# Earlier and regrouped loads of q, k and v at the start of a kernel of attention and two MLPs

## The reference

```python
scores = cap * np.tanh(scale * (q @ k.T) / cap)
attn = np.exp(scores - max(scores)); attn = attn / (attn.sum() + 1e-9)
x = (attn @ v) reshaped to (896, 768)
x = square(relu(x @ w_in1)) @ w_out1        # w_in: 768 x 2048, w_out: 2048 x 768
x = silu(x @ w_in2) @ w_out2
```

## Time and profile before

| | |
|---|---|
| median of 3 runs | 555.83 us (555.57 to 556.46) |
| the profiled execution | 555.52 us, span 553.7 us |
| mean granted TensorE clock | 0.992 |
| PE busy | 537.8 us, 97% |
| DVE busy | 387.5 us, 70% |
| ACT busy | 258.9 us, 47% |
| POOL busy | 82.2 us, 15% |
| DMA | 42.16 MB, mean 76 GB/s |

### The profile page before, as it was taken

The page is one execution under the profiler, slowest core; times in us unless marked ns, Lnnn a source line. Parts: engine busy times, 40 slices in busy tenths (PEclk is TensorE's granted clock), DMA queues, the critical chain, the costliest instruction groups (busy, mean ns, idle before and its releaser), DMA issues.

```text
span 553.7 us, 7148 instructions
## 1 busy us (share of the span) xinstructions
PE 537.8 (97%) x2636; PEld 443.3 (80%) x2636; DVE 387.5 (70%) x621; ACT 258.9 (47%) x397; POOL 82.2 (15%) x54
## 2 busy tenths in 40 slices
PE   7999999999999999999999999999999999999994
PEld 5333333799988999999889999999999999998993
DVE  2189999977779653677799845556965255569983
ACT  3988889054444322444444444454432244443330
POOL 0989999300000000000000000000000000000000
PEclk9899999999999999999999999999999999999997
DMA  6679740151202202422012124111220141112544
GB/s 156 167 204 223 190 118 2 56 134 57 57 21 71 63 1 57 134 59 57 19 47 54 35 59 133 58 29 49 65 69 2 57 134 57 51 27 61 84 61 73
DMA packets 82372, 42.16 MB, mean 76 GB/s; under 512 B 27040, under 2 KB 79264, under 8 KB 82336
## 3 DMA queue, kind: packets, MB, share of 16 engines
q1 hardware_dynamic: 81184, 41.12, 28.8%
q10 hardware_dynamic: 1120, 0.57, 0.5%
q0 software_dynamic: 32, 0.00, 0.0%
HBM read 38.93 MB, written 2.75 MB: 75 GB/s over the span
## 4 chain that ended last, share of the span: by engine, by line
PE 84%; DVE 5%; SPq 3%; ACT 3%; DMA 1%; issue 1%; ACTq 0%; DVEq 0%
PE banks L486 25%; PE banks L488 24%; PE banks L487 24%; PE banks L444 5%; PE banks L433 3%; SPq L300 2%; DVE w_hl L838 2%; PE banks L452 2%; DMA qk_raw<-in_q_dram 1%; PE banks L430 1%; ACT g_hi L671 1%; SPq L318 1%; DVE y L918 1%; ACT prob L588 1%; DVE g_lo L879 1%
## 5 line engine op out<-in xcount | busy, mean ns | idle before, releaser
L486 PE MATMUL banks<-x_hi,w_hl 128*128 128x448 f32 x384 | 140.7, 367 | 0.0
L488 PE MATMUL banks<-x_hi,w_hl 128*128 128x448 f32 x384 | 140.5, 366 | 0.0
L487 PE MATMUL banks<-x_lo,w_hl 128*128 128x448 f32 x384 | 140.5, 366 | 0.0
L486 PE MATMUL banks<-g_hi,w_hl 128*128 128x448 f32 x336 | 123.5, 368 | 2.6 <-DVE w_hl L838 2.5
L488 PE MATMUL banks<-g_hi,w_hl 128*128 128x448 f32 x336 | 122.9, 366 | 0.0
L487 PE MATMUL banks<-g_lo,w_hl 128*128 128x448 f32 x336 | 122.9, 366 | 0.0
L486 PEld LDWEIGHTS banks<-x_hi,w_hl 128*128 128x128 f32 x384 | 72.1, 188 | 7.6 <-issue 1.4
L488 PEld LDWEIGHTS banks<-x_hi,w_hl 128*128 128x128 f32 x384 | 72.1, 188 | 6.2
L487 PEld LDWEIGHTS banks<-x_lo,w_hl 128*128 128x128 f32 x384 | 72.1, 188 | 6.2
L833 DVE TENSOR_TENSOR w_hl<-w_raw,w_hl 128x768 fp32r<-128x768 f32 x32 | 32.5, 1016 | 55.1 <-ACT w_hl L620 55.0
L486 PEld LDWEIGHTS banks<-g_hi,w_hl 128*128 128x128 f32 x336 | 63.1, 188 | 9.8 <-DVE w_hl L838 4.5
(11 more groups left out here) (67 smaller groups left out, 562.5 us busy)
## 6 DMA issues: line engine op xcount, KB each, us to landing
w_raw<-in_moe_w_in_dram SPq DMA_DIRECT2D x32, 384.0 KB, 3.4
w_raw<-in_moe_w_out_dram SPq DMA_DIRECT2D x24, 512.0 KB, 5.3
qk_raw<-in_k_dram SPq DMA_DIRECT2D x48, 112.0 KB, 2.5
qk_raw<-in_q_dram SPq DMA_DIRECT2D x44, 112.0 KB, 2.7
out_dram<-rows SPq DMA_DIRECT2D x46, 56.0 KB, 2.2
v_t<-in_v_dram SPq DMA_DIRECT2D x24, 96.0 KB, 2.7
qk_raw<-in_q_dram ACTq DMA_DIRECT2D x4, 112.0 KB, 4.4
v_x<-in_v_dram SPq DMA_DIRECT2D x24, 16.0 KB, 1.9
```

The costliest lines, as they stand in the source:

```text
L486: pe.matmul(dst, hi[:, kk, :], mov_hi, start=start, stop=False)
L487: pe.matmul(dst, hi[:, kk, :], mov_lo, start=False, stop=False)
L488: return pe.matmul(dst, lo[:, kk, :], mov_hi, start=False, stop=stop)
```

## The change

SP no longer waits for pair 0's loads: pair 1's k and q are issued right behind pair 0's k. The quarter rows of v are loaded for all 12 pairs at once, by four DMAs of 96 KB with the same runs of 256 bytes, issued behind pair 1, on a semaphore of their own that TensorE waits on ahead of pair 0's output. The first main part of v (four DMAs into `v_t`) is issued by ACT behind its four q loads; SP still issues the other five parts in their places.

```diff
         s_v_in = [sem(f"s_v_in{i}") for i in range(len(V_PARTS) - 1)]
+        s_v_x_in = sem("s_v_x_in")
...
+
+            def load_v_x():
                 for h in range(2):
                     for g in range(XB):
                         at = (MB + g) * D
                         rp = slice(D * h + BL * g, D * h + BL * g + BL)
-                        sp.dma_start(v_x[rp, first:last, h, :],
-                                     v_rest[h, :, first:last, at:at + D]).then_inc(s_v_in[part], DMA)
+                        sp.dma_start(v_x[rp, :, h, :], v_rest[h, :, :, at:at + D]).then_inc(s_v_x_in, DMA)
...
             load_part(At(0, 0), 0, k_v, s_first_in[0])
-            for n in range(2):
-                sp.wait_ge(s_first_in[n], 4 * DMA)
             load_qk(At(0, 1))
-            load_v(0)
+            load_v_x()
...
                 if j.n in V_PARTS:
-                    pe.wait_ge(s_v_in[V_PARTS.index(j.n)], 8 * DMA)
+                    pe.wait_ge(s_v_in[V_PARTS.index(j.n)], 4 * DMA)
+                if j.n == 0:
+                    pe.wait_ge(s_v_x_in, 2 * XB * DMA)
...
                     act.dma_start(qk_raw[0][rp, at:at + QB * D], q_v[0, h]).then_inc(s_first_in[1], DMA)
+            for g in range(C):
+                at = g * CW * D
+                act.dma_start(v_t[BL * g:BL * g + BL, 0:2 * V_PARTS[1], :],
+                              v_main[:, 0:2 * V_PARTS[1], at:at + CW * D]).then_inc(s_v_in[0], DMA)
```

## The result

The changed kernel takes 555.16 us (median of 22 runs, 553.55 to 556.26), the kernel before beside it 556.39 us (22 runs, 554.47 to 557.88). The ratio is 0.9978, with a 95% interval of 0.9968 to 0.9988: 1.2 us faster, with 0.7 to 1.8 us in the interval. That lies in the forecast range (554.1 to 556.2 us, 555.05 us the likeliest). The forecast reckoned 0.78 us of gain from the median of 555.83 us of three runs; on 22 runs that median is 556.39 us. So it is partly luck that 555.05 us lies so near to 555.16 us: the base was 0.56 us too low, and the gain 0.44 us too small.

The account below looks back on a forecast made before the run. SP's issue time up to pair 3's loads was taken to bound the start, then TensorE, with ACT second. 0.20 us (pair 1's start) and 0.58 us (pair 3) make 0.78 us off 555.83 us: 555.05 us, range 554.1 to 556.2 us.

Parts of the forecast that it names:

- What bounds the start: Start of kernel: SP's issues up to pair 3's last load, then TensorE; gain is what pair 3's scores move from 30.55 us.
- Pair 1 by bytes: Pair 1's loads: bytes, not issues, set their arrival; landing at 13.1 us, 0.2 us earlier, between 12.8 and 13.6 us.
- a pair 1 with no v_t in its way: Pair 1's loads if SP's queue came first: in at 11.8 us, 1.0 us before the early end of 12.8 us.
- Pair 0 at 8.8 us: TensorE's first scores: pair 0's still start at 8.8 us; if not, loads are mixing.
- mixing in full: Pair 0's loads sharing engines with pair 1's and v's: scores 5.7 us later, 560.1 us; the slower case had 0.10.
- The clock falls again (0.45): TensorE at pair 1's scores: half clock from about 15.6 to 19.0 us; 0.78 us of gain, 555.05 us.
- the rival that it stays (0.27): TensorE at pair 1: clock stays at 2.4 GHz, ACT limits; 1.45 us of gain, 554.4 us; chance 0.27.
- ACT's limit for pair 3: Pair 2's fourth score block waits for ACT's first tanh until 24.3 us, so pair 3's scores start at 29.1 us at best.
- v_x and v_t at no cost after pair 3: After pair 3 SP is off the chain: 24 issues, 11 us of its time over 70 us, cost nothing.
- Does the gain last: Near 95 us: GpSimd has 1.5 us of slack, so 0.78 us fits and 1.45 us just so; DVE gains slack.
- The size: Whole kernel: 0.20 us from pair 1's start plus 0.58 us at pair 3, 0.78 us of gain.

Follow-up runs that it names:

- the two pairs of parts that were run: Changed kernel with SP's wait on pair 0's loads put back: ratio 0.9983; changed kernel with v's first part issued by SP, not ACT: 0.9978.
- the last run: Kernel before with SP waiting for the cap's load, not pair 0's, v_x merged behind v's first part on SP, 17 warm-up matmuls; ratio 0.9956.
- the run with the filler: Kernel before with ten extra warm-up matmuls on TensorE between the scores of pair 0 and those of pair 1; ratio 0.9993.

## Why the prediction was right, and where it was right by luck

**What bounds the start: right.** SP's issues set pair 3, and pair 3 set the rest. With the wait alone taken out the whole gain is there, the two pairs of parts that were run come within 0.1% of it, and the distance from pair 3's scores to the first MLP matmul is 66.5 us before and after (97.09 - 30.55, 96.19 - 29.67).

**Pair 1 by bytes: right, 0.36 us off.** 13.46 us against 13.1 us, in its bounds of 12.8 to 13.6 us. The share of v_t was forecast as the reason; without v_t on ACT's queue pair 1 came at 11.22 and 11.47 us, even earlier than the 11.8 us that the forecast had for a pair 1 with no v_t in its way.

**Pair 0 at 8.8 us: wrong.** This step failed. Its scores began at 9.67 us, 0.88 us late. The forecast had named mixed loads as the only cause that could make them late. The mixing was real, but small. In the five kernels in which nothing is issued behind pair 0 until its loads are in, or nearly so, its first transpose starts at 7.23 to 7.34 us; with loads of pair 1 or v_t at once behind it, at 7.70 to 8.03 us; in the last run, at 7.53 us. The forecast had 5.7 us for mixing in full. The mixing didn't set the start of the scores, either. Where pair 0's scores wait for DVE they follow the first transpose by 1.31 to 1.32 us, so that 7.75 us would have let them begin at some 9.06 us (an estimate). What held them until 9.67 us is the warm-up, which I had not put into the sum at all: 22 matmuls end at 8.86 us in the profile of before and at 9.74 us after, and the scores wait for them in both. This later end does not need the change: the run with the filler, where nothing differs from before up to this point, has it at 9.91 us, and the run with v_x alone, with pair 0 turned from 7.23 us, at 9.74 us. Without pair 3's late load behind it, this scatter is no longer hidden, and a part of the gain hangs on it from execution to execution.

**The clock falls again (0.45): wrong;** the rival that it stays (0.27) came true in its condition, but not at its price of 1.45 us of gain, since pair 0 was late. The two misses nearly cancelled, which is luck. ACT's chain gave 22.41 us for pair 2 where the forecast, by way of a slow clock, had 22.5 us, and 29.67 us for pair 3 where it had 29.77 us. A late pair 0 seems even to help the clock here, for it shortens the idle time ahead of pair 1, but no run shows this apart from the rest. Over all profiles of this case the clock fell where this idle time was 2.32, 2.45, 2.61 and 2.65 us, and stayed at 1.00 where it was 1.95 us or less. In the changed kernel's 22 runs the mean clock was 0.994 or less in three and 0.996 or more in 16, so there the clock mostly stayed up.

**ACT's limit for pair 3: mis-sized.** I had pair 3 at best at 29.1 us, 20.3 us behind pair 0's scores. Where nothing else held it, it came 20.0 us behind (29.67 - 9.67), as its fourth block does not wait for ACT in pair 2 (22.41 + 2.45 = 24.86 us, where it starts).

**v_x and v_t at no cost after pair 3: right** for SP's time. For the start, the move of v_t to ACT is a loss by itself (pair 0 and pair 1 both later), and it only pays by the issues it takes from SP.

**Does the gain last: right for this change, with less to spare than I saw.** I put 1.5 us of slack on GpSimd and called DVE safe. GpSimd's block took 3.22 us instead of 2.66 us and ended at 95.24 us for sums at 95.30 us. DVE had 0.15 us to spare before, which is far less than the gain; it gained slack, as forecast, by starting `finish(0)` at 26.78 us and not at 30.41 us, and has 0.49 us to spare after. Where pair 3 was turned late, a start 1 us earlier still was taken back by DVE.

**The size.** 0.78 us were forecast and 0.90 us measured in the profiles at the end of attention, 1.2 us in the timed runs. The interval of these holds both. A part of the rest may be pair 4's idle time, which the profile of before does not have and the run with the filler has, and a part that the profile of before is of a fast execution; no run here counts how often either comes.

## What to carry to other kernels

Where a queue's issues are the bound, count them up to the transfer that is waited for, and take out the wait that keeps them back before regrouping anything: one deleted wait gave what three edits gave. An earlier load helps only until the next bound, here ACT's chain behind the very first scores; so look at once what starts that chain, warm-up matmuls among it, because a warm-up that ends late, which a late load used to hide, is then on the path. And a step that comes out right should be checked by its parts, since a late start and a clock that stayed up cancelled here.

## What the runs showed of the hardware

**The warm-up ends at different times.** The same 22 matmuls took 6.67 us in the profile of before, 7.55 us after and 6.75 to 7.72 us in the others. The column of the granted clock says 1.00 all through, but the number of matmul records in 1.5 us nearly doubles at some point, near 5.5 us before and only near 7 us after. First before, then after:

```profile
4.00:5.50 1.50, 1.50 (x10) 1.50 (x9) 0.01 (x1) 0.00 (x0) 0.00 (x0) 1.00 0.97 223
5.50:7.00 1.50, 1.50 (x16) 1.50 (x15) 0.62 (x4) 0.62 (x1) 0.00 (x0) 1.00 0.31 57
```

```profile
5.50:7.00 1.50, 1.50 (x9) 1.50 (x8) 0.55 (x4) 0.70 (x1) 0.00 (x0) 1.00 0.99 234
7.00:8.50 1.50, 1.50 (x15) 1.50 (x14) 0.75 (x2) 0.79 (x2) 0.00 (x0) 1.00 1.12 227
```

The clock record that is kept with each trace, and that no view prints, says what this is. It has no entry ahead of 5.34 us before and ahead of 7.25 us after, where it begins with the full clock; the column counts a time without an entry as 1.00. Over the eight profiles with 22 warm-up matmuls the first entry lies between 5.34 and 7.61 us, and the later it lies, the later the warm-up ends (8.86 to 9.91 us). So this is the step from 1.2 to 2.4 GHz, by half the pace ahead of it, and it scatters from execution to execution; no row gives the lower level itself.

**Two paces of the same matmuls.** In each of the four stages of the MLPs' second products, 60 matmuls in a row take either 12.16 us or 12.40 us, for the whole stage, whichever kernel it is. The same two matmuls, 60 apart, in the third such stage, first before (12.16 us), then after (12.40 us):

```profile
397.30 0.36 PE L486 MATMUL banks<-g_hi,w_hl 128*128 128x448 f32 x1
...
409.46 0.36 PE L486 MATMUL banks<-g_hi,w_hl 128*128 128x448 f32 x1
```

```profile
396.70 0.37 PE L488 MATMUL banks<-g_hi,w_hl 128*128 128x448 f32 x1
...
409.10 0.37 PE L488 MATMUL banks<-g_hi,w_hl 128*128 128x448 f32 x1
```

From the first to the last matmul of the MLPs it is 447.4 to 447.5 us with no slow stage (2 profiles), 448.2 to 448.5 us with one (6), 449.0 to 449.3 us with two (6). That is 0.8 us a stage, and up to 1.8 us between two of these profiles, where the runs of one kernel scatter over about 3 us. The two profiles of the result have one slow stage each, so it doesn't explain the difference between them. What picks the pace is not shown.
